# Banded attention scores masked, reduced and shifted inside their PSUM banks

## What is computed

```python
q_d = q.reshape(B, H, Sd, factor, D).mean(axis=3)      # factor = 4; k_d, v_d alike
out_up = np.repeat(sm_attn(q_d, k_d, v_d), factor, axis=2)
mask = np.abs(pos[:, None] - pos[None, :]) < factor
scores = np.where(mask, scale * np.matmul(q, k.transpose(0, 1, 3, 2)), -1000000000.0)
scores = scores - np.max(scores, axis=-1, keepdims=True)
attn = np.exp(scores)
attn = attn / (np.sum(attn, axis=-1, keepdims=True) + 1e-09)
x = heads_side_by_side(out_up + np.matmul(attn, v))    # 2304 x 512
x = leaky_relu(x @ w_in1, 0.01) @ w_out1               # d_ff = 2048
h = x @ w_in2; return (h - np.tanh(h)) @ w_out2
```

## Time and profile before

| what | before |
|---|---|
| median of 3 runs | 975.35 us (973.09 to 975.36) |
| the profiled execution, time | 973.22 us |
| its span in the profile | 971.4 us |
| PE (matmul) busy | 945.4 us, 97% of the span, 6960 instructions |
| DVE busy | 548.4 us, 56%, 1074 instructions |
| ACT busy | 559.9 us, 58% |
| POOL busy | 405.3 us, 42% |

### The profile page before, as it was taken

How to read it: one execution, slowest core, us unless ns; L and a number is a source line. 1 busy time by engine, 2 the same in 40 slices (tenths; PEclk the granted TensorE clock), 3 DMA queues, 4 the chain that set the end, 5 groups by cost and what they waited for, 6 DMA issues and landing times.

```text
span 971.4 us, 19773 instructions
## 1 busy us (share of the span) xinstructions
PE 945.4 (97%) x6960; PEld 887.2 (91%) x6960; DVE 548.4 (56%) x1074; ACT 559.9 (58%) x1355; POOL 405.3 (42%) x343
## 2 busy tenths in 40 slices
PE   6798999999999999999999999999999999999998
PEld 6688999999999999999999998799889899898996
DVE  5753454455445635544335576776676666766764
ACT  4645544545546446455355777676665665656754
POOL 1755724616418236255261846532233233333232
PEclk9979999999999999999999999999999999999999
DMA  6963222112211220112002212000000000000000
GB/s 141 206 188 87 54 49 51 27 24 50 49 26 24 50 50 24 26 27 66 1 2 68 74 45 86 13 33 1 27 6 1 32 0 0 32 0 0 33 1 33
DMA packets 87797, 41.48 MB, mean 43 GB/s; under 512 B 60352, under 2 KB 81344, under 8 KB 87744
## 3 DMA queue, kind: packets, MB, share of 16 engines
q1 hardware_dynamic: 87744, 40.78, 16.2%
HBM read 36.04 MB, written 4.72 MB: 42 GB/s over the span
## 4 chain that ended last, share of the span: by engine, by line
PE 82%; POOL 7%; ACT 4%; issue 3%; DVE 2%; DMA 2%; SPq 0%; ACTq 0%; POOLq 0%; DVEq 0%
PE ph L511 12%; PE ph L512 12%; PE ph L513 12%; PE acc L587 6%; PE acc L540 6%; PE acc L588 6%; PE acc L589 6%; PE acc L541 6%; PE acc L542 6%; PE banks L409 2%; PE banks L441 2%; PE banks L428 2%; POOL in_lo L1038 1%; POOL g_lo L1059 1%; POOL w_lo_b L1066 1%
## 5 line engine op out<-in xcount | busy, mean ns | idle before, releaser
L1059 POOL TENSOR_TENSOR g_lo<-scratch,g_hi 128x384 fp32r<-128x384 f32 x96 | 126.2, 1314 | 258.5 <-ACT g_hi L696 258.5
L917 DVE TENSOR_TENSOR ph<-g,ph 128x288 f32<-128x288 f32 x128 | 58.9, 461 | 165.5 <-ACT g L710 164.9
L511 PE MATMUL ph<-x_hi,w_hi_a 128*128 128x288 f32 (+1 forms) x448 | 144.9, 323 | 1.4 <-DVE x_lo L899 0.8
L512 PE MATMUL ph<-x_lo,w_hi_a 128*128 128x288 f32 (+1 forms) x448 | 141.0, 315 | 0.0
L513 PE MATMUL ph<-x_hi,w_lo_a 128*128 128x288 f32 (+1 forms) x448 | 140.9, 315 | 0.0
L1038 POOL TENSOR_TENSOR in_lo<-w_whole,in_hi 128x512 fp32r<-128x512 f32 x64 | 84.6, 1322 | 132.3 <-ACT in_hi L680 132.3
L710 ACT ACTIVATE g<-ph 128x288 f32<-128x288 f32 x128 | 52.5, 410 | 133.1 <-PE ph L513 133.1
L951 DVE SCALAR_TENSOR_TENSOR scratch<-scratch,ph 128x384 f32<-128x384 f32 x96 | 53.2, 554 | 111.7 <-ACT scratch L759 107.1
L1043 POOL TENSOR_TENSOR out_lo<-w_whole,out_hi 128x512 fp32r<-128x512 f32 x64 | 86.1, 1345 | 71.9 <-ACT out_hi L684 71.7
L758 ACT ACTIVATE scratch<-ph 128x384 f32<-128x384 f32 x96 | 46.8, 487 | 108.4 <-PE ph L513 106.8
L904 DVE TENSOR_TENSOR g_lo<-ph,g_hi 128x288 fp32r<-128x288 f32 x128 | 58.6, 458 | 59.2 <-ACT g_hi L696 59.2
(11 more groups left out here) (260 smaller groups left out, 2668.5 us busy)
## 6 DMA issues: line engine op xcount, KB each, us to landing
out_dram<-o_stage SPq DMA_DIRECT2D x18, 256.0 KB, 2.1
w_whole<-in_moe_w_in_dram SPq DMA_DIRECT2D x16, 256.0 KB, 3.8
w_whole<-in_moe_w_out_dram SPq DMA_DIRECT2D x16, 256.0 KB, 4.2
qn<-in_q_dram SPq DMA_DIRECT2D x26, 144.0 KB
kn<-in_k_dram SPq DMA_DIRECT2D x26, 144.0 KB
v4n<-in_v_dram SPq DMA_DIRECT2D x26, 144.0 KB
vw<-in_v_dram SPq DMA_DIRECT2D x26, 122.5 KB
scratch<-in_moe_w_in_dram SPq DMA_DIRECT2D x8, 256.0 KB, 2.8
```

Source lines behind the costliest of these rows:

```text
L511: pe.matmul(bank, whi, x_hi[:, c, 0:width], start=(c == 0), stop=False)
L512: pe.matmul(bank, whi, x_lo[:, c, 0:width], start=False, stop=False)
L917: dve.tensor_tensor(ph1[:, f % 2, 0:T1], g1[:, f % 2, :], ph1[:, f % 2, 0:T1], ALU.max)\
L1059: pool.tensor_tensor(g2_lo[:, f % 3, :], g2[:, f % 2, :], g2_hi[:, f % 3, :].bitcast(F32), ALU.subtract).then_inc(g_lo_done, 1)
```

## The change

The mask is added in place, in the PSUM bank. The maximum is taken per bank, from PSUM, and the subtraction reads the bank and writes `pl`. Two DVE instructions (maximum, subtraction of 630 columns each) become four (350 and 280 columns each), and both masks write PSUM in place of SBUF. `bank_free[0]` is now set by the subtraction of bank 0, which stands in step 5, and `bank_free[1]` by the subtraction of bank 1, for which ACT's exponential now waits. The diff:

```diff
--- before.py
+++ after.py
@@ -161,8 +161,9 @@
                 self.bank_free = [sem(f"bank_free0_{which}"), sem(f"bank_free1_{which}")]
                 self.q_loaded, self.k_loaded = sem(f"q_loaded_{which}"), sem(f"k_loaded_{which}")
                 self.v_loaded = sem(f"v_loaded_{which}")
+                self.masked_l = sem(f"masked_l_{which}")
                 self.max_l, self.max_d = sem(f"max_l_{which}"), sem(f"max_d_{which}")
-                self.means_done, self.sub_l = sem(f"means_done_{which}"), sem(f"sub_l_{which}")
+                self.means_done = sem(f"means_done_{which}")
                 self.exp_l, self.sum_l = sem(f"exp_l_{which}"), sem(f"sum_l_{which}")
                 self.eps_l, self.eps_d = sem(f"eps_l_{which}"), sem(f"eps_d_{which}")
                 self.inv_l, self.inv_d = sem(f"inv_l_{which}"), sem(f"inv_d_{which}")
@@ -634,7 +635,7 @@
                     act.wait_ge(s.bank_full[0], uses0(i, 2))
                     act.activation(k_part(s, 1), tokens(s, 1), ACT.Copy, scale=K_SCALE).then_inc(s.bank_free[0], 1)
                 elif step == 7:
-                    act.wait_ge(s.sub_l, i + 1)
+                    act.wait_ge(s.bank_free[1], uses1(i, 3))
                     act.activation(s.pl[:, :, :], s.pl[:, :, :], ACT.Exp, scale=L_SCALE).then_inc(s.exp_l, 1)
                 elif step == 8:
                     act.wait_ge(s.max_d, i + 1)
@@ -839,6 +840,13 @@
                     src.rearrange("p (m f) -> p m f", f=FACTOR),
                     s.up[:, m0:m1].rearrange("p (m o) -> p m o", o=1).to_broadcast([P, m1 - m0, FACTOR]), ALU.add)
 
+            def local_scores(s, bank):
+                n0, n1 = (0, NBA) if bank == 0 else (NBA, NB)
+                return s.banks[:, bank, 0:(n1 - n0) * WIN].rearrange("p (n w) -> p n w", w=WIN)
+
+            def maxima(s, n0, n1):
+                return s.mxl[:, n0:n1].rearrange("p (n o) -> p n o", o=1).to_broadcast([P, n1 - n0, WIN])
+
             def attention(step, s, i, batch, c):
 
                 if step == 3:
@@ -852,20 +860,24 @@
                     last.then_inc(s.means_done, 1)
                 elif step == 4:
                     dve.wait_ge(s.bank_full[0], uses0(i, 3))
-                    src = s.banks[:, 0, 0:NBA * WIN].rearrange("p (n w) -> p n w", w=WIN)
-                    dve.tensor_tensor(s.pl[:, 0:NBA, :], src, band[:, 0:NBA, :], ALU.add).then_inc(s.bank_free[0], 1)
+                    masked = local_scores(s, 0)
+                    dve.tensor_tensor(masked, masked, band[:, 0:NBA, :], ALU.add).then_inc(s.masked_l, 1)
                     dve.tensor_reduce(s.kdT[:, :], s.kT[:, PAD:PAD + S].rearrange("p (t f) -> p t f", f=FACTOR),
                                       AX_X, ALU.add).then_inc(s.means_done, 1)
+                    dve.wait_ge(s.masked_l, 2 * i + 1)
+                    dve.tensor_reduce(s.mxl[:, 0:NBA], masked, AX_X, ALU.max).then_inc(s.max_l, 1)
                 elif step == 5:
                     dve.wait_ge(s.bank_full[1], uses1(i, 3))
-                    src = s.banks[:, 1, 0:(NB - NBA) * WIN].rearrange("p (n w) -> p n w", w=WIN)
-                    dve.tensor_tensor(s.pl[:, NBA:NB, :], src, band[:, NBA:NB, :], ALU.add).then_inc(s.bank_free[1], 1)
-                    dve.wait_ge(s.bank_free[1], uses1(i, 3))
-                    dve.tensor_reduce(s.mxl[:, :], s.pl[:, :, :], AX_X, ALU.max).then_inc(s.max_l, 1)
-                    dve.wait_ge(s.max_l, i + 1)
-                    dve.tensor_tensor(s.pl[:, :, :], s.pl[:, :, :],
-                                      s.mxl[:, :].rearrange("p (n o) -> p n o", o=1).to_broadcast([P, NB, WIN]),
-                                      ALU.subtract).then_inc(s.sub_l, 1)
+                    masked = local_scores(s, 1)
+                    dve.tensor_tensor(masked, masked, band[:, NBA:NB, :], ALU.add).then_inc(s.masked_l, 1)
+                    dve.wait_ge(s.max_l, 2 * i + 1)
+                    dve.tensor_tensor(s.pl[:, 0:NBA, :], local_scores(s, 0), maxima(s, 0, NBA), ALU.subtract)\
+                        .then_inc(s.bank_free[0], 1)
+                    dve.wait_ge(s.masked_l, 2 * i + 2)
+                    dve.tensor_reduce(s.mxl[:, NBA:NB], masked, AX_X, ALU.max).then_inc(s.max_l, 1)
+                    dve.wait_ge(s.max_l, 2 * i + 2)
+                    dve.tensor_tensor(s.pl[:, NBA:NB, :], masked, maxima(s, NBA, NB), ALU.subtract)\
+                        .then_inc(s.bank_free[1], 1)
                 elif step == 7:
                     dve.wait_ge(s.bank_full[0], uses0(i, 4))
                     quarter = s.banks[0:QP, 0, 0:QT * SD_].rearrange("p (t k) -> p t k", t=QT)
```

## The result

| | before | after |
|---|---|---|
| median | 975.18 us (973.09 to 975.36, 5 runs) | 978.96 us (978.71 to 981.11, 5 runs) |
| profiled execution, time and span | 973.22, 971.4 us | 978.71, 976.9 us |
| layer 1's first matmul | 53.70 us | 64.07 us |
| from there to the first L428 (L429 after) | 21.69 us | 19.46 us |

The ratio is 1.0053 with a 95% interval of 1.0036 to 1.0070: the medians are 3.8 us apart, where I had forecast 0.7 us and "no difference" as the likeliest. The time lies inside the range that I gave; the case that came is the first rival.

A forecast was written before the change was run, and what follows sets the result against it. PE was taken as the bound from 100 to 440 us. First batch +5.2, start of layer 1 -4.6 and later pairs +0.1 gave +0.7 us on 975.35: 976.0 us, with 8 in 10 from 972.8 to 980.0.

The forecast's parts named there:

- the first rival: First batch costs more than layer 1 gives, TensorE's clock falling or returning late: +3.9 us, 979.2 us; chance 0.22.
- What bounds the kernel: From 100 to 440 us PE is busy 338.18 of 340.00 us; DVE edits matter there only if PE waits.
- The instructions at about nothing: DVE's mask, maximum and subtraction work per pair: 3.15 us before, 3.19 after, +0.04 us; PSUM no dearer than SBUF.
- The first batch at +5.2 us: Pairs a to d: bank 0 freed later, PE waits at L476, delays carry on; layer 1 starts at 58.9 us.
- 0.4 us for its later rise in pair c's scores: First batch, pair c: the clock rises during the scores, adding 0.4 of the 1.28 us.
- my upper bound of 6.6: First batch: no waits for ACT go and pair c's scores run at half clock throughout; lower bound 3.7 us.
- The start of layer 1 at -4.6 us: Layer 1's first subtraction no longer stalls behind POOL, 2.83 us, plus 1.75 for the clock; bounds 2.8 to 5.5.
- The second half of it, 1.75 us for the clock: Start of layer 1: PE's wait shrinks, so the half-clock stretch from 75.50 to 78.90 us should go.
- The later pairs at +0.1 us: Later pairs: L476 still finds bank 0 free, by 0.09 us; bounds 1.0 us dearer to 0.6 us less.
- The sum: Whole kernel: 5.2 - 4.6 + 0.1 = +0.7 us on the median of 975.35, giving 976.0 us.
- The new subtraction waits for POOL too: Rival: still waits through its SBUF output or the maxima, nothing gained in layer 1; 980.7 us, chance 0.06.
- That PSUM costs more: Rival: PSUM costs 0.06 us more an instruction, +0.7 + 1.0, about 977.0 us; chance 0.10.

The follow-up runs named there:

- split in SBUF: Against the changed kernel: maximum and subtraction still split by bank, but masks write the SBUF tile and subtractions have both inputs in SBUF; 981.96 us, 1.0101 of before.
- the extra matmuls: Changed kernel plus 3, 7, 11 and 11 unused matmuls in PE's waits for bank 0 at pairs a to d; 972.46 us, 1.0006 of before.
- the two second traces: Both kernels run again unchanged: before 972.75 us at the median, layer 1 starting at 55.72; after 979.38 us, layer 1 starting at 65.53.
- the second trace of before: The kernel before, run again unchanged: the traced run took 972.07 us, layer 1 began at 55.72; median 972.75 us, ratio 1.0004.
- the second group: Group of runs with all waits filled, the split in SBUF and both unchanged kernels again; the changed kernel took 979.38 us, before beside it 973.38.
- the kernel with the earlier subtraction: Against the changed kernel, only the subtraction of bank 0 moved from step 5 to the end of step 4; 975.22 us, 1.0028 of before.

## Why the prediction was wrong

- **What bounds the kernel** held: between 100 and 440 us PE was busy for 338.2 us before and 338.5 after, and what the change did, it did before 100 us.
- **The instructions at about nothing** held: 3.14 us from the mask to DVE's next work where I had 3.19. An instruction that reads PSUM was hardly dearer: the maximum over 350 columns took 515 ns from a bank (after) and 508 from `pl` (split in SBUF), the subtraction of 280 columns 451 ns from a bank and 451 from `pl` where it was not held up. The figures of the Trainium skill that I weighed against it (by my estimate from them 65 ns more each, "VectorE: DVE Perf Modes", section on the TRN2 errata) did not show here.
- **The first batch at +5.2 us** is where it failed. Its chain was right, with each wait, its place and its cause; with the clock kept by the extra matmuls it gives 4.5 us (up to 5.8 if the early rise in pair b's scores is not counted). But I took one change of the clock into it, 0.4 us for its later rise in pair c's scores, and carried the rest of the clock's course over from before. The waits that I had worked out myself were long enough to bring the clock down again: it fell 5.4 us earlier (42.8, for 48.2), and came back 11.7 us later (70.1, for 58.4). That stretch covers all of the batch's end, and there the forecast failed most: up to pair d's L477 the delay was +6.9 us (42.32 for 35.42) where I had 5.9, and from there to layer 1 I had it shrink by 0.7 us, where it grew by 3.5 (21.75 us for 18.28). The term measured +10.4 (+9.8 between the two second traces), twice its size, and stands above my upper bound of 6.6, which had allowed for half clock in pair c's scores alone. I had the mechanism only as a sentence in the first rival, unpriced at the place where it acted, and the argument that I set against it, that PE mostly waits for others in the first batch, was wrong for a half clock: PE was busy for 18.72 of 21.10 us.
- **The start of layer 1 at -4.6 us** was right in mechanism and near in size. Two traces with the same start and the same course of the clock up to there compare it cleanly: before (53.70) and the version that changes only layer 1 (53.54) need 21.69 and 18.84 us to the first L428, 2.85 us less for 2.83 forecast; the half-clock stretch behind it is gone as well. In the medians it gave 3.3 and 4.5 us. The second half of it, 1.75 us for the clock, is not certain: in the second trace of before the clock did not fall there. In the changed kernel itself this stage gave 2.2 us up to L429, as it began with 6 us at half clock for 4.7, and 3.8 us up to the scores of layer 1's second pair (104.17 for 97.63, after a start 10.4 us late).
- **The later pairs at +0.1 us** held: PE's list of waits has DVE's L874 four times, all in the first batch. L477 followed the mask by 142.34 - 139.77 = 2.57 us at the pair that answers to the earlier trace rows, still without a wait.
- **The sum** lies inside my range partly by luck. With the first batch at 10.4 my own terms give 10.4 - 4.6 + 0.1 = +5.9, 981.2 us, which is outside it. By the traces the kernel was 6.5 us behind at the scores of layer 1's second pair and 5.5 us in span; the medians are 3.8 us apart in these runs and 6.0 in the second group (979.38 for 973.38). Behind 100 us two traces of the kernel before itself differ by 1.5 us.
- **The rivals.** The first came true in its mechanism, with 10.4 in place of 6.6, and a gain of 3.8 in place of 2.8. "The new subtraction waits for POOL too" is ruled out by its 0.51 us in the middle of POOL's L1027. That PSUM costs more is ruled out above.

What stays open: what exactly decides whether the clock falls after a given wait. Waits of 1.57 and 1.77 us were followed by it, one of 1.75 us did no more than leave the clock low, and of two waits of 2.81 us in the same place one was followed by it and one was not. In the second trace of before it fell between 45.4 and 46 us, in the middle of work, 1.5 us after a wait of 1.19. Why POOL is later in the later pairs of the kernel with the earlier subtraction is open as well.

## What to carry to other kernels

When an instruction that frees a buffer is moved, follow what the waiting engine has queued behind that wait, and after that ask whether the wait is on TensorE: idle times of 1 to 2 us there can cost more than their length, because what follows can run at half clock for long (27 us here, and up to 5.9 of the 10.4 us lost). Price that on the whole stage that follows, as a case of its own. A change can be good in one stage and bad in another; taking it only where it pays (here the pairs inside layer 1) gave 0.3 to 0.4% where the whole change lost 0.5 to 0.75%. And where GpSimd works without pause beside VectorE, keep one input of an elementwise instruction of two inputs in PSUM: here it did not get caught behind GpSimd then (0.51 us for 3.68).

## What the runs showed of the hardware

- A VectorE instruction with two inputs in SBUF can stand still while GpSimd runs an instruction on SBUF: 3.68 and 3.55 us for 630 columns that take 0.82 otherwise, 2.85 us for 280 columns that take 0.45. With one of its two inputs in PSUM it ran through (0.51 and 0.45 us), and so did the reductions, with one input (0.43 us for 280 columns beside POOL's L1026); but a `tensor_scalar` of 96x3 is held up as well (L897 after the change: 0.87 us from 81.43, ended with POOL's L1045 at 82.28; 0.15 where it is not held, 0.87 at the median of the thirteen pairs in buffers a). The Trainium skill has this ("SBUF — State Buffer", section "Who interferes with whom"): two SBUF inputs contend with GpSimd's reads, reductions do not contend on this chip, and `tensor_scalar` can. What I had not expected is that splitting one such instruction into two cost 8.6 us over the kernel (981.96 for 973.38).
- 32 matmuls that nobody reads, placed in TensorE's waits, made a kernel 6.9 us faster; 23 of them at the end of the first batch made another 2.8 us faster (966.31 for 969.09).
- The same kernel scatters by 10 us from run to run (969 to 979 us for before). Its two traces differ by 2 us in the start of layer 1, with the scores of one pair at 1.70 us in one and 2.99 in the other, that is at either level of the clock.
